# Turning the next slot's rows earlier, and one half of relu between two quarters of new weights

## What is computed

```python
logits = x @ w_gate + modality_bias[modality_id]
e_idx = np.argmax(logits, axis=1)
...
for e in range(E):
    mask = e_idx == e
    if not mask.any():
        continue
    h = np.maximum(x[mask] @ w1[e], 0.0)
    out[mask] = gate_w[mask, None] * (h @ w2[e])
```

## Time and profile before

| | us |
|---|---|
| median of 3 runs | 896.7 (896.53 to 897.51) |
| profiled execution, its own time | 895.34 |
| span of the profiled execution | 893.6 |
| TensorE busy in it | 854.3 |
| attention and routing, up to slot 0 | 0 to 397.7 |
| slots 0 to 6 | 397.7 to 490.7 |
| second mixture | 491.3 to 893.6 |

### The profile page before, as it was taken

The page is one execution under the profiler, slowest core; times in us unless marked ns, Lnnn a source line. Parts: engine busy times, 40 slices in busy tenths (PEclk is TensorE's granted clock), DMA queues, the critical chain, the costliest instruction groups (busy, mean ns, idle before and its releaser), DMA issues.

```text
span 893.6 us, 13581 instructions
## 1 busy us (share of the span) xinstructions
PE 854.3 (96%) x4884; PEld 714.9 (80%) x4884; DVE 545.6 (61%) x1083; ACT 341.9 (38%) x726; POOL 301.5 (34%) x253
## 2 busy tenths in 40 slices
PE   7799999967999999989999999999999999999998
PEld 6588888855676766657777999899898999899886
DVE  5999999999999999963562542342141422332111
ACT  5455656544765656533654322222030311122010
POOL 7976767657676869512111300000000000000000
PEclk9599999996999999999999999999999999999999
DMA  9320000032354554137390700211011200000001
GB/s 205 104 95 13 25 13 13 14 133 88 123 207 135 213 159 143 65 121 268 135 321 34 271 1 1 95 39 57 0 48 48 94 0 0 0 0 0 35 23 47
DMA packets 49394, 75.60 MB, mean 85 GB/s; under 512 B 24624, under 2 KB 24624, under 8 KB 49328
## 3 DMA queue, kind: packets, MB, share of 16 engines
q1 hardware_dynamic: 43088, 60.62, 20.0%
q0 software_dynamic: 4160, 13.63, 5.0%
q10 hardware_dynamic: 2080, 0.52, 0.3%
HBM read 63.49 MB, written 11.27 MB: 84 GB/s over the span
## 4 chain that ended last, share of the span: by engine, by line
PE 54%; DVE 40%; issue 3%; ACT 2%; DMA 1%; ACTq 0%; SPq 0%; DVEq 0%
DVE work L1141 18%; PE bank L1558 17%; PE bank L1560 17%; PE bank L1559 17%; DVE top L1146 14%; DVE top L1132 5%; PE bank L1553 2%; ACT w2h L922 1%; ACT w1h L922 1%; DMA k_raw<-in_k_dram 1%; PE bank L1619 0%; DVE kTl L1093 0%; DVE w2l L1383 0%; DVE den L1159 0%; DVE x_cur L1174 0%
## 5 line engine op out<-in xcount | busy, mean ns | idle before, releaser
L1146 DVE MAX8 top<-work 128x8 f32<-128x576 f32 x216 | 152.3, 743 | 0.0
L681 POOL TENSOR_SCALAR att<-sc,top 128x576 f32<-128x576 f32 x70 | 120.8, 1726 | 81.2 <-DVE top L1146 80.5
L1495 DVE SCALAR_TENSOR_TENSOR hT<-bank,hT 128x384 fp32r<-128x384 f32 x96 | 52.7, 557 | 126.1 <-ACT hT L1044 125.7
L1558 PE MATMUL bank<-xT,w1h 128*128 128x384 f32 x384 | 128.8, 335 | 0.6 <-issue 0.6
L1560 PE MATMUL bank<-xT,w1h 128*128 128x384 f32 x384 | 128.4, 334 | 0.0
L1559 PE MATMUL bank<-xT,w1l 128*128 128x384 f32 x384 | 128.3, 334 | 0.0
L1044 ACT ACTIVATE hT<-bank 128x384 fp32r<-128x384 f32 x96 | 46.9, 492 | 194.5 <-PE bank L1560 194.5
L1560 PE MATMUL bank<-w2l,hT 128*128 128x512 f32 x288 | 112.2, 390 | 0.0
L1559 PE MATMUL bank<-w2h,hT 128*128 128x512 f32 x288 | 112.2, 390 | 0.0
L1558 PE MATMUL bank<-w2h,hT 128*128 128x512 f32 x288 | 112.1, 389 | 0.0
L1141 DVE MATCH_REPLACE8 work<-top,work 128x576 f32<-128x576 f32 x144 | 106.4, 744 | 0.0
(11 more groups left out here) (278 smaller groups left out, 1447.5 us busy)
## 6 DMA issues: line engine op xcount, KB each, us to landing
w_raw<-in_moe_w_dram SPq DMA_DIRECT2D x92, 512.0 KB, 6.1
q_raw<-in_q_dram SPq DMA_DIRECT2D x18, 128.0 KB, 3.2
v_one<-in_v_dram POOLq DMA_DIRECT2D x18, 128.0 KB, 5.1
out_dram<-x_tok SPq DMA_DIRECT2D x9, 256.0 KB, 2.0
y_dram<-zero POOLq DMA_DIRECT2D x2, 1024.0 KB, 6.7
w_early<-in_moe_w_dram SPq DMA_DIRECT2D x4, 512.0 KB, 7.9
y_dram<-b_ys POOLq DMA_DIRECT2D x7, 256.0 KB, 5.3
k_raw<-in_k_dram SPq DMA_DIRECT2D x6, 256.0 KB, 5.1
```

What stands on the lines that cost most here:

```text
L681: nc.gpsimd.tensor_scalar(att[:, g % ATR, :], sc[:, g % RING, :], top8[:, g % RING, 3, 7:8], None, ALU.is_ge).then_inc(keep_made, 1)
L1146: nxt = nc.vector.max(out=top8[:, g % RING, i + 1, :], in_=work[:, j, :])
L1495: nc.vector.scalar_tensor_tensor(out=hTl(b)[:, f, :], in0=bank[:, HB + f % 4, 0:BW], scalar=0.0, in1=f32(hTh(b)[:, f, :]), op0=ALU.max, op ...
L1558: nc.tensor.matmul(dst, high_lhs, high_rhs, start=start, stop=False)
```

## The change

On TensorE, `turn_slot(s + 1)` and, in slots 3 to 5, `x_transposes` move from behind the second half of rows times w1 to right behind `turn_hidden(0)`, ahead of the half's step c = 2. On ScalarE, with a new expert, the relu of half 0 moves from behind the fourth quarter of w2 to ahead of it; without one it is in the Else branch, with the same waits.

```diff
+            def slot_relu_half(s, i):
+                act.wait_ge(slot_h, 2 * s + i + 1)
+                if s >= 1:
+                    act.wait_ge(slot_hT, 2 * s - 1 + i)
+                nc.scalar.activation(b_hs[:, i * 512:(i + 1) * 512], bank[:, HB + i, :], ACT.Relu).then_inc(slot_relu, 1)
...
                         act.wait_ge(slot_y, s)
-                        split_high(kth, w2_raw, w2h, w2_loaded, w2_high)
+                        split_high(kth, w2_raw, w2h, w2_loaded, w2_high, (0, 1, 2))
+                        slot_relu_half(s, 0)
+                        split_high(kth, w2_raw, w2h, w2_loaded, w2_high, (3,))
+                    with act.Else():
+                        slot_relu_half(s, 0)
                 for i in range(2):
-                    act.wait_ge(slot_h, 2 * s + i + 1)
-                    if s >= 1:
-                        act.wait_ge(slot_hT, 2 * s - 1 + i)
-                    nc.scalar.activation(b_hs[:, i * 512:(i + 1) * 512], bank[:, HB + i, :], ACT.Relu).then_inc(slot_relu, 1)
+                    if i == 1 or s == 0:
+                        slot_relu_half(s, i)
...
                             turn_hidden(0)
+                            turn_slot(s + 1)
+                            if GA.tiles <= s < 2 * GA.tiles:
+                                x_transposes(s - GA.tiles)
                         last = product(bank[:, HB + i, :], b_xsTh[:, c, :], b_xsTl[:, c, :], w1h[:, c, i * 512:(i + 1) * 512],
                                        w1l[:, c, i * 512:(i + 1) * 512], c == 0, c == DC - 1)
                     last.then_inc(slot_h, 1)
-                turn_slot(s + 1)
-                if GA.tiles <= s < 2 * GA.tiles:
-                    x_transposes(s - GA.tiles)
```

## The result

| | before | after |
|---|---|---|
| median of 12 runs, us | 896.68 | 898.62 |
| lowest to highest | 895.21 to 898.49 | 896.41 to 899.68 |
| profiled execution, its own time | 895.34 | 898.42 |
| its span | 893.6 | 896.7 |

The ratio is 1.0022, with a 95% interval of 1.0013 to 1.0031: the change costs about 2.0 us (1.2 to 2.8). The forecast was 897.4 us, 0.7 slower, with a range up to 898.8; the measured median lies near that upper end.

A forecast was written before the change was run, and what follows sets the result against it. The prediction took TensorE as the bound, busy for 854.3 of 893.6 us. It summed -0.76 (relu waits) and +1.47 (gather wait) to +0.7 us on the median 896.7, giving 897.4 us, range 895.6 to 898.8.

The forecast's parts named there:

- The ScalarE edit in slots 3 and 4, -0.76: Slots 3 and 4: TensorE's wait for relu of half 0 goes whole, 0.38 us in each.
- the second rival: Half 0's low part or ScalarE's branch replaces the relu wait; the 0.76 is lost, 898.2 us; chance 0.1.
- The order of blocks on TensorE, 0: Where rows are there, the moved transposes cost the same in either place: 0, between -0.1 and +0.1 us per slot.
- The wait for the gather in slot 1, +1.47: Slot 1: moved `turn_slot(2)` still waits for slot 2's rows until 416.63, delaying f = 0 by 1.47 us.
- The first rival: Slot 1: slot 2's rows land before 415.05 in most executions, leaving only the gain, 895.9 us; chance 0.17.
- "I cost it at nothing", of the Else branch: Slots that keep their expert: ScalarE's 6.06 us idle ahead of relu covers the Else branch, cost 0.
- Sum: -0.76 + 1.47 = +0.7 us, put on the median 896.7, gives 897.4 us; chance 0.65.
- The clock, third rival: Slot 1's new 1.6 us pause lowers TensorE's clock, costing 1.7 us more: 899.1 us; chance 0.08.

The follow-up runs named there:

- the change in slots 1 to 5: Changed kernel with ScalarE's moved relu in slots 1 to 5 only: 1.0015 of the kernel before; with ScalarE's never-run slot 13 code also left out, 0.9996.
- the run with one Else: Kernel before plus one Else branch of three semaphore increments on ScalarE, in slot 1 only: ratio 1.0019.
- run with the change in slots 1 to 5 and slot 13 out: Changed kernel with the moved relu in slots 1 to 5 only and ScalarE's never-run code for slot 13 left out: 0.9996 of the kernel before.
- the 13 increments: Kernel before plus 13 semaphore increments on ScalarE ahead of slot 0, no branch: ratio 1.0026; with ScalarE's slot 13 code also left out, 0.9989.
- the best version: Kernel before with relu moved in slots 1 to 5, ScalarE's slot 13 code left out, slot 2's gather issued earlier, TensorE unchanged: ratio 0.9991.

## Why the prediction was right, and where it was not

**The result lay in the range, and slower as forecast, but the largest term of it, 2.0 us, is one that the prediction costed at nothing.** That the time came out slower at all is luck: with the pause away, the change in slots 1 to 5 measures 0.9996 of the kernel before (0.9982 to 1.0010).

- *The ScalarE edit in slots 3 and 4, -0.76.* Right: 0.37 and 0.43 in the changed kernel, within 0.1 us of that in the four other kernels that have it. VectorE's low part, the next in line, did not get in the way, so the second rival didn't come. Slot 4's share scatters more than one pair of profiles shows: without the edit the slot takes 14.31 to 14.80 us in nine profiles (a wait for relu of 0.20 to 0.45 in seven, none over 0.1 in two), with it 14.14 to 14.21 in five; the means lie 0.44 apart.
- *The order of blocks on TensorE, 0.* Right: slots 2, 5 and 6 of both runs of the TensorE edit alone are as long as before to 0.11 us. It gains nothing either, in any slot.
- *The wait for the gather in slot 1, +1.47.* The mechanism is right and its size was read from one execution. In the 12 profiles in which GpSimd issues the gather late, it lands 15.5 to 19.9 us behind the start of slot 0, by issue and landing time of each. The moved transposes want the rows at 17.4, where slot 0 ran at full clock; the old ones at 18.9. Before's 18.85 was the second latest of the twelve; the latest, 19.94 in the run with one Else, was late even for the old place, so that its slot 1 took 13.85. The wait was 1.26 and 0.85, and slot 1 longer by 1.4 and 1.0, in the two profiles of the moved transposes that had a late landing and full clock; it was nothing in the third at full clock (landed at 16.5), and nothing in the changed kernel's own profile, where slot 0 took 2.6 us longer and hid it. Worked out from the 12 landings, the wait at full clock is 0.76 us on the mean and that of the old place 0.09 (0.97 and 0.12 from the nine whose slot 0 ran at full clock). So the term is an estimate of +0.7 to +0.85 in place of +1.47, and less in the executions with a slow slot 0; timed by itself, the TensorE edit costs 0.6 us (-0.4 to 1.7). The first rival, a gather in time, is thus what happens in a part of the executions.
- *"I cost it at nothing", of the Else branch.* **This is the step that failed.** The idle 6.06 us that was to cover it is ahead of each slot's relu; the price falls behind the last slot, where ScalarE jumps over the code of the slots that aren't there. It has 2.07 us of pause; TensorE is later by 1.20 in slot 6 and by 0.83 behind it, +2.0 in all. No rival held it: that instructions can cost time by where they put the code behind them was not thought of.
- *Sum.* -0.8 + 2.0 + up to 0.85 gives +1.2 to +2.1, against a measured 2.0 (1.2 to 2.8).
- *The clock, third rival.* With the pause of 1.26 us in slot 1 (run with the change in slots 1 to 5 and slot 13 out) the clock stayed at 2.4 GHz:

```profile
412.00:416.00 4.00, 2.74 (x16) 2.10 (x15) 0.69 (x1) 1.20 (x2) 0.00 (x0) 1.00 1.01 292
416.00:420.00 4.00, 4.00 (x23) 3.37 (x22) 0.69 (x1) 1.43 (x3) 1.00 (x1) 1.00 1.04 404
```

The time came near that rival's 899.1 by another way. But what the rival feared does occur at the other pause: in two of the seven kernels with ScalarE's pause (the ScalarE edit alone and the 13 increments), TensorE's clock falls behind its own pause of 2.04 and 1.78 us, and the stretch to the end takes 403.8 in place of 403.0. The other five, with 1.78 to 1.96 us, keep the clock. From the first of the two:

```profile
494.00:496.00 2.00, 2.00 (x8) 2.00 (x7) 2.00 (x3) 2.00 (x3) 0.58 (x1) 0.50 0.10 43
```

What is shown and what isn't: that the pause depends on where the code lies is shown, in seven kernels that have it (4 to 52 more instructions than before) and by taking it away from two of them (the 13 increments, and the change in slots 1 to 5) by leaving out code that never runs. That it falls at the jump is shown by the trace's record of the branch itself (line 422): in the changed kernel it stands at 487.37 and ScalarE's next instruction at 489.85; before, at 486.33 and 486.76. That distance is 2.46 to 2.72 us in the seven kernels with the pause and 0.43 in the seven profiles without. That it is a fetch of instructions is a reading. The Trainium skill (Runtime: NRT & Kernel Launch, Instruction fetch mechanics) states it: an engine other than TensorE streams its instructions in blocks of 256 and holds two of them, and a taken branch whose target is in neither waits until a DMA has fetched it. The runs agree in that the pause is a step, of 2.05 to 2.31 us, and comes at a jump; in which block a given instruction lies is not known here. That rule spoke against the change, and the prediction should have had it as a rival of the Else branch.

Of the best version only so much can be said: from slot 0's first matmul to the end it takes 893.8 - 398.65 = 495.15 us in its profile, before 893.6 - 397.72 = 495.88, so 0.7 less; its ratio to the kernel before is 0.9991 with an interval that reaches 1.0004. It beats the kernel before by its slots, not yet by its times; 0.18 of what it gains is lost in its slot 6, and why is open. Against the changed kernel, by their ratios to the kernel before, it is about 2.8 us faster; the two were not timed side by side.

## What to carry to other kernels

Where an engine jumps over code that isn't needed, every instruction added to it anywhere ahead can move the jump's target over an edge such as the one here, and the price falls at the jump and not at the edit: look at the first instruction behind each long jump for an "issue" pause, and drop code that cannot run before adding any. A transfer that lands just in time in one profile is no constant: take several landings relative to the stage before moving its reader, or issue it as soon as its buffer is free, which here was 10 us earlier and showed no cost.

## What the runs showed of the hardware that was not expected

- 4, 12 or 44 more instructions on ScalarE, branch or no branch, give the same pause of 2.07 or 2.08 us at the jump behind the last slot, and 12 or 15 fewer give none.
- VectorE has a pause at its own jump behind the last slot in all 14 profiles, the kernel before included: 2.81 to 3.13 us from the branch to its next instruction, with no wait between (before: 486.97 to 490.02). There it costs nothing, as VectorE then waits for GpSimd's low part (ready at 490.5). No run moved VectorE's code, so whether it is the same thing isn't shown.
- The granted clock fell to 1.2 GHz in slot 0 in four of 14 executions, behind a pause that they all have; it costs up to 2.6 us there. The prediction's argument from one profile that such a pause leaves the clock alone (1.00 from 393.5 to 397.5) was too strong, though it held for the pause in slot 1; behind the last slot a pause of TensorE of 1.8 to 2.0 us went with a fallen clock in two profiles of seven, 0.8 us each.
- The same gather takes 5.3 to 9.9 us from issue to landing here. The Trainium skill (DMA: Bandwidth & Descriptors, Anatomy of one DMA) would give 2.6 us, an estimate; no gather of slot 2's rows came near it, not even the one issued at 396.42 (5.3 us).
